# The first expert mixture in rounds of 416 moving tokens, with pieces of the weights stationary

## The reference

```python
x = attention(q, k, v)                         # local window of 16 and block summaries
# first mixture: two experts for each token
noisy = x @ w_gate + log1p(exp(x @ w_noise)) * noise
top2 = the two largest of noisy; top2_w = softmax over the two
for e in range(8):
    out[mask] += top2_w * (relu(x[mask] @ w1[e]) @ w2[e])
# second mixture: tokens with x @ w_skip > 0 get one expert; out = x + gate * expert(x)
```

## Time and profile before

| | us |
|---|---|
| median of 3 runs | 760.32 |
| lowest and highest | 758.58, 762.24 |
| the profiled execution | 759.18 |
| its span, from the first to the last instruction | 757.3 |
| PE busy with products and turns | 661.1 |
| DVE busy | 383.0 |
| ACT busy | 311.6 |
| POOL busy | 188.4 |

### The profile page before, as it was taken

The page is one execution under the profiler, slowest core; times in us unless marked ns, Lnnn a source line. Parts: engine busy times, 40 slices in busy tenths (PEclk is TensorE's granted clock), DMA queues, the critical chain, the costliest instruction groups (busy, mean ns, idle before and its releaser), DMA issues.

```text
span 757.3 us, 13865 instructions
## 1 busy us (share of the span) xinstructions
PE 661.1 (87%) x3940; PEld 533.5 (70%) x3940; DVE 383.0 (51%) x753; ACT 311.6 (41%) x512; POOL 188.4 (25%) x236
## 2 busy tenths in 40 slices
PE   5787884499999999999999999949399979999794
PEld 5676763387878878878788787836277768777583
DVE  2774787545454436254344363611655567447621
ACT  2364662144444334244343444414054465545511
POOL 1537750112222222222222222210012212212321
PEclk8898995599999999999999999988679998999997
DMA  9999993154656536447274456556436667557211
GB/s 196 212 223 250 247 345 115 32 161 128 177 130 176 129 88 163 99 125 181 43 181 125 99 156 150 155 121 189 119 129 185 210 217 232 174 173 251 41 41 15
DMA packets 94911, 117.12 MB, mean 155 GB/s; under 512 B 55380, under 2 KB 55508, under 8 KB 94864
## 3 DMA queue, kind: packets, MB, share of 16 engines
q1 hardware_dynamic: 77408, 91.10, 41.5%
q0 software_dynamic: 10528, 24.81, 17.2%
q10 hardware_dynamic: 6928, 0.66, 0.7%
HBM read 99.90 MB, written 20.98 MB: 160 GB/s over the span
## 4 chain that ended last, share of the span: by engine, by line
PE 61%; DMA 16%; SPq 8%; issue 6%; DVE 5%; POOLq 1%; ACT 1%; POOL 1%; ACTq 0%; DVEq 0%
PE bank L723 47%; DMA xg<-x_moe,ix_take 7%; DMA out<-y_sb,ix_put 6%; SPq L432 5%; PE bank L739 4%; PE bank L695 2%; SPq L447 2%; PE bank L644 1%; PE bank L622 1%; DVE col_val L1284 1%; PE bank L634 1%; PE bank L605 1%; PE bank L808 1%; DMA late_raw<-in_q 1%; PE bank L594 1%
## 5 line engine op out<-in xcount | busy, mean ns | idle before, releaser
L723 PE MATMUL bank<-w_hi,xt_hi 128*128 128x512 f32 x336 | 140.0, 417 | 16.1 <-DVE w_lo L1169 7.9
L1169 DVE TENSOR_TENSOR w_lo<-stage,w_hi x120 | 142.3, 1222 | 18.7 <-ACT w_hi L847 14.5
L1349 DVE TENSOR_TENSOR ht_lo<-bank,ht_hi 128x512 fp32r<-128x512 f32 x84 | 58.0, 691 | 168.2 <-ACT ht_hi L948 166.4
L723 PE MATMUL bank<-w_hi,ht_hi 128*128 128x512 f32 x336 | 139.7, 416 | 0.0
L723 PE MATMUL bank<-w_lo,xt_hi 128*128 128x512 f32 x336 | 135.1, 402 | 0.0
L723 PE MATMUL bank<-w_lo,ht_hi 128*128 128x512 f32 x336 | 131.8, 392 | 0.0
L847 ACT CAST w_hi<-stage x120 | 120.8, 1050 | 25.4 <-PEq L765 23.0
L945 ACT ACTIVATE h_sb<-bank 128x512 f32<-128x512 f32 x84 | 50.3, 598 | 113.5 <-PE bank L723 107.9
L723 PE MATMUL bank<-w_hi,xt_lo 128*128 128x512 f32 x336 | 93.1, 400 | 0.0
L948 ACT CAST ht_hi<-bank 128x512 fp32r<-128x512 f32 x84 | 49.3, 587 | 102.3 <-PE bank L739 102.3
L723 PE MATMUL bank<-w_hi,ht_lo 128*128 128x512 f32 x336 | 91.0, 393 | 0.0
(11 more groups left out here) (124 smaller groups left out, 703.7 us busy)
## 6 DMA issues: line engine op xcount, KB each, us to landing
stage<-in_moe_w SPq DMA_DIRECT2D x128, 512.0 KB
v_win<-in_v SPq DMA_DIRECT2D x24, 192.0 KB, 6.6
x_moe<-zeros SPq DMA_DIRECT2D x13, 260.0 KB, 4.1
x_att<-x_sb POOLq DMA_DIRECT2D x12, 256.0 KB, 5.2
x_sb<-x_moe SPq DMA_DIRECT2D x12, 256.0 KB, 2.7
out<-x_moe SPq DMA_DIRECT2D x4, 768.0 KB, 8.7
late_raw<-in_v SPq DMA_DIRECT2D x6, 384.0 KB, 7.3
stage<-in_k SPq DMA_DIRECT2D x6, 256.0 KB, 6.8
```

The source lines that it names most:

```text
L723: last = eng.matmul(ps[:], *every[i], start=(i == 0), stop=(i == len(every) - 1))
L1169: eng.tensor_tensor(piece(w_lo[n % SETS], j), stage[:, j, :], piece(w_hi[n % SETS], j).bitcast(F32), ALU.subtract)\
L1349: eng.tensor_tensor(ht_lo[:, half].rearrange("p k n -> p (k n)"), ps_ht[half][:], ht_hi[:, half].bitcast(F32).rearrange("p k n -> p (k n)" ...
```

## The change

The first mixture gets code of its own (`first_mixture` on each engine); the second keeps the slots (now `second_mixture`). The operands of the first change places: pieces of 128x128 of the weights are stationary, and the tokens, turned, move, up to 416 at a time. A *round* is 416 tokens of one expert in four parts of 128, 128, 128 and 32 rows, and with the counts above each expert has one round. The hidden layer comes out with the hidden units on the partitions, so that it needs no turn; the output comes out with its columns on the partitions and is turned back, in four chunks of 128 columns. The middle layer is made in two halves of four units of 128 ("units"); after each half its share of the output is added to four PSUM banks (`ps_out`). A round has 8 x 12 products for the units and 2 x 4 x 12 for the output. In the second half PE also turns the next round's x and, one chunk late, the output; the last chunk is turned behind unit 1 of the next round.

ACT has one instruction for a unit (relu and rounding at once), DVE one (relu of PSUM less the rounded part). POOL issues four gathers without waiting between them, PE waits for each by a semaphore of its own; and four scatters, whose landings are awaited together. A scatter leaves rows past the expert's count out, where they went to spare rows before. The table of pieces is `ROUND_PIECES`. `NBLK` grows from 12 to 16 (four rounds of four parts), with it `take_ix`, `put_ix`, `over` and `column_h` of both routings; the first routing has two more instructions, and the lists count rounds. Constants are loaded in two DMAs, and many tiles lie in other places: those of the routing, of the slots and of the rounds share memory.

```diff
+PART = (P, P, P, P // 4)
+PSTART = (0, P, 2 * P, 3 * P)
+W = sum(PART)
+PARTS = len(PART)
+ROUNDS = -(-N // W)
+NBLK = PARTS * ROUNDS
...
-SLOT_PIECES = ((2, 0, 1, 0), (2, 1, 2, 3))
+ROUND_PIECES = (0, 1, 0, 1, 0, 1, 0, 1, 1, 1, 1, 1)
+SLOT_PIECES = (2, 1, 2, 3)
...
+def block_starts(m):
+    b = np.arange(NBLK)
+    return b // PARTS * W + np.array(PSTART)[b % PARTS] if m == 0 else P * b
...
+            def first_mixture():
+                S = round_sems
+                eng.sem_inc(S["xtp"], 1)
+                def turn_x(n, t, ps):
+                    rows = PART[t]
+                    for i in range(DK):
+                        last = eng.transpose(ps[:, i * rows:(i + 1) * rows],
+                                             rows_in[0:rows, t, i * P:(i + 1) * P],
+                                             ident[0:rows, 0:rows])
+                    last.then_inc(S["xtp"], 1)
+                def turn_y(n, chunk):
+                    eng.wait_ge(S["yt"], n * DK + (chunk + 4))
+                    eng.wait_ge(S["ye"], n * DK + (chunk + 1))
+                    for t in range(PARTS):
+                        last = eng.transpose(ps_turn[0:PART[t], t * P:(t + 1) * P],
+                                             out_t[:, PSTART[t]:PSTART[t] + PART[t]], ident)
+                    last.then_inc(S["ytp"], 1)
+                def units(n, f, hi, lo):
+                    eng.wait_ge(S["hte"], n * FK + (f + 1))
+                    half, at = divmod(f * P, D)
+                    mine = [(w[:, FH * i + half, at:at + P], x[:, i, :])
+                            for x, ws in ((tok_hi, (hi, lo)), (tok_lo, (hi,)))
+                            for i in range(DK) for w in ws]
+                    for i, (w, x) in enumerate(mine):
+                        last = eng.matmul(ps_unit[f % 2][:, 0:W], w, x, start=(i == 0),
+                                          stop=(i == len(mine) - 1))
+                    last.then_inc(S["h"], 1)
+                def columns(f, chunk, hi, lo):
+                    for i, (w, h) in enumerate(((hi, unit_hi), (lo, unit_hi), (hi, unit_lo))):
+                        last = eng.matmul(ps_out[chunk][:, 0:W],
+                                          w[:, WC // 2 + f, chunk * P:(chunk + 1) * P],
+                                          h[:, f % UNITS, :], start=(f == 0 and i == 0),
+                                          stop=(f == FK - 1 and i == 2))
+                    return last
+                def one_round(e):
+                    hi, lo = w_hi[e % SETS], w_lo[e % SETS]
+                    n = eng.snap(number, min_val=0, max_val=E * ROUNDS)
+                    eng.wait_ge(S["xth"], n * PARTS + PARTS)
+                    eng.wait_ge(S["xte"], n * PARTS + (PARTS + 1))
+                    for part in range(FK // UNITS):
+                        mine = range(part * UNITS, (part + 1) * UNITS)
+                        for f in mine:
+                            units(n, f, hi, lo)
+                            if f == 1:
+                                turn_y(n, 0)
+                        if part == 0:
+                            if e == 0:
+                                eng.wait_ge(s_first, PIECES)
+                            else:
+                                eng.wait_ge(s_lo, PIECES * e)
+                        for chunk in range(DK):
+                            if part == 0:
+                                eng.wait_ge(S["yt"], n * DK + (chunk + 1))
+                            for i, f in enumerate(mine):
+                                if chunk == 0 and i >= UNITS - 2:
+                                    eng.wait_ge(S["hth"], n * FK + (f + 1))
+                                    eng.wait_ge(S["hte"], n * FK + (f + 3))
+                                if part and i == 2 and chunk:
+                                    turn_y(n, chunk)
+                                if part and i == 1:
+                                    eng.wait_ge(s_take[chunk], (n + 2) * 16)
+                                    eng.wait_ge(S["xte"], n * PARTS + (PARTS + chunk + 1))
+                                last = columns(f, chunk, hi, lo)
+                                if part and i == 1:
+                                    turn_x(n + 1, chunk, ps_x)
+                            if part:
+                                last.then_inc(S["y"], 1)
+                    eng.reg_add(number, number, 1)
+                    eng.reg_add(done, done, 1)
+                eng.wait_ge(s_route, 1)
+                eng.reg_load(counts, todo_i[0:1, 0:E])
+                for t in range(PARTS):
+                    eng.wait_ge(s_take[t], 16)
+                    turn_x(0, t, ps_out[t])
+                for e in range(E):
+                    if e == 0:
+                        eng.wait_ge(s_first, PIECES // 2)
+                    else:
+                        eng.wait_ge(s_lo, PIECES * e - PIECES // 2)
+                    eng.reg_mov(done, 0)
+                    with eng.While(lambda: eng.snap(done) < eng.snap(counts[e])):
+                        one_round(e)
+                    eng.drain().then_inc(s_wfree, 1)
+                turn_y(eng.snap(number, min_val=0, max_val=E * ROUNDS), 0)
...
+                def one_round(e):
+                    n = eng.snap(number, min_val=0, max_val=E * ROUNDS)
+                    for part in range(FK // UNITS):
+                        for f in range(part * UNITS, (part + 1) * UNITS):
+                            eng.wait_ge(S["h"], n * FK + (f + 1))
+                            eng.activation(unit_hi[:, f % UNITS, :], ps_unit[f % 2][:, 0:W], ACT.Relu)\
+                               .then_inc(S["hth"], 1)
+                            round_next(e + 1, f)
+                        for chunk in range(DK):
+                            if part == 0:
+                                round_next(e + 1, FK + chunk)
+                                continue
+                            round_x(n + 1, chunk, ps_x)
+                            eng.wait_ge(S["y"], n * DK + (chunk + 1))
+                            eng.wait_ge(S["ytp"], n * DK + (chunk + 1))
+                            eng.copy(out_t[:], ps_out[chunk][:, 0:W]).then_inc(S["yt"], 1)
...
+                def take(n, e, blocks):
+                    eng.wait_ge(S["xtp"], n * PARTS + 1)
+                    eng.sem_inc(S["start"], 1)
+                    eng.tensor_copy(ix_take[:], take_ix[:, e, blocks]).then_inc(S["ixt"], 1)
+                    eng.wait_ge(S["ixt"], n + 1)
+                    eng.wait_ge(S["gate"], n + 1)
+                    eng.sem_inc(S["start"], 1)
+                    for t in range(PARTS):
+                        rows = PART[t]
+                        eng.indirect_dma_start(rows_in[0:rows, t, :], None, x_dram,
+                                               bass.IndirectOffsetOnAxis(ap=ix_take[0:rows, t:t + 1],
+                                                                         axis=0),
+                                               bounds_check=N - 1).then_inc(s_take[t], 16)
+                def put():
+                    n = eng.snap(sent, min_val=0, max_val=E * ROUNDS)
+                    eng.wait_ge(S["ye"], n * DK + (DK + 2))
+                    eng.wait_ge(S["ix"], n + 1)
+                    eng.sem_inc(S["start"], 1)
+                    for t in range(PARTS):
+                        rows = PART[t]
+                        eng.indirect_dma_start(x1_dram,
+                                               bass.IndirectOffsetOnAxis(ap=ix_put[0:rows, t:t + 1],
+                                                                         axis=0),
+                                               rows_out[0:rows, t, :], None, bounds_check=N - 1,
+                                               oob_is_err=False, compute_op=ALU.add).then_inc(s_put[t], 16)
+                    for t in range(PARTS):
+                        eng.wait_ge(s_put[t], n * 16 + 16)
+                    eng.sem_inc(S["yfree"], 1)
...
+                        dv = eng.snap(done, min_val=0, max_val=ROUNDS - 1)
+                        take(round_now(), e, bass.ds(dv * PARTS, PARTS))
+                        with eng.If(round_now() >= 2):
+                            put()
...
+                if m == 0:
+                    eng.tensor_reduce(round_f[:, mine, tiles],
+                                      over[:, mine, tiles, PARTS - 1:NBLK - 1:PARTS], AX.X, ALU.add)
...
+                if m == 0:
+                    near = near_f
+                    then(eng.scalar_tensor_tensor(near_f[:, mine, tiles], round_f[:, mine, tiles],
+                                                  float(PARTS * P - W), rank_f[:, mine, tiles],
+                                                  ALU.mult, ALU.add))
...
-                then(eng.tensor_scalar(count_i[:], count[:], float(P - 1), None, ALU.add))
-                then(eng.tensor_scalar(nblk_i[:], count_i[:], 7, None, ALU.arith_shift_right))
+                if m == 0:
```

(104 more changed lines are left out.)

322 lines of the change are left out of this document (217 added, 105 removed).

## The result

The changed kernel takes 750.73 us, the median of 4 runs (747.26 to 752.08), and the kernel before 759.45 (757.31 to 762.24). The ratio is 0.9876 with a 95% interval of 0.9828 to 0.9924: faster by 1.2%, or 8.7 us. The forecast was 750, within 741 to 760, and 10.3 us less than before. The profiled execution took 752.08 us, with a span of 750.3.

What follows compares the result with a forecast made beforehand. PE at its upper clock was taken to bound the first mixture. PE's sequence -26.0, waits +5.2, head +4.3, tail +5.7 and second routing +0.5 gave -10.3 us: a median of 750 us, range 741 to 760.

Steps and rivals of the forecast that it cites:

- head: Before the first mixture: longer routing, four gather issues and a small last part delay PE's first product; +4.3 us.
- the wait at ps_x: Behind unit 7, DVE's queued work makes PE stand 0.65 us a round for that one buffer; +5.2 us in all.
- tail: Behind the first mixture's last product: last chunk's turns and scaling, then three scatters ahead of the last; +5.7 us.
- PE's sequence: First mixture on PE without new waits: 1536 products at 0.190 us plus turns, 327.7 us against 353.7; -26.0 us.
- rival (a): First mixture: weight load becomes the bound, no product faster than 0.22 us; 46 us on top, 796 us; 8%.
- point of decision: First mixture: from 0.1967 us a product on, the load-bound case decides, the forecast gain of 10.3 us being used up.
- Rival (b): First mixture: weight loads overlap no product, so 192 additional loads show 0.11 us each; 21 us more, 771 us; 2%.
- The expert's end: PE's stop between experts in the first mixture, carried over unchanged at 0.89 us for each of seven ends.
- The cover that held: Within rounds, one round of PE hides gather and scatter, some 7 and 11 us each if exposed; unit remainders in time.
- (c): Within a round, one covered item is late too, 1 us a round or so: 8 us, 758 us; 18%.
- (d): First mixture: each loop body's some 450 PE instructions run once; 762 us if each round lost 1.5 us; 4%.
- (e): More gain: 0.187 us a product with better overlapping scatters and gathers, or no ps_x wait; 741 to 745 us; 13%.

Runs made afterwards that it cites:

- the run of half products: Against the changed kernel, each middle-layer product of 416 columns issued as two of 208 with the same weights, each with its own load; 762.82 us, one run.

## Why the prediction was right, step by step

The terms, with what the two profiles show in their places (us):

| | forecast | profiles |
|---|---|---|
| up to the routing | 0 | -0.8 |
| head, from the routing to the first product | +4.3 | +5.3 |
| first mixture on PE, with the wait at ps_x | -20.8 | -21.1 |
| tail, to the last landing | +5.7 | +5.8 |
| from there to the second mixture | +0.5 | +0.4 |
| second mixture | 0 | +3.5 |
| sum (of unrounded terms) | -10.3 | -7.0 |

So the first mixture and what stands around it were forecast within 1.0 us a term. The second mixture was not; about 2 of its 3.5 us were that one execution. That the median lies within 0.7 us of 750 is in part luck: it fell by 8.7 us and not 10.3, and the kernel before was 0.9 faster in these runs than in those from which the forecast started.

**PE's sequence** (-26.0 forecast, -20.8 with the wait). The columns and a fixed part gave 0.190 us; the trace has 0.189, and the run with 404 columns 0.183 to 0.184. The groups of turns cost the 0.44 us that was carried over. The choice that mattered was to leave the weight load out as a bound; the run of half products shows what it is, 0.11 us, as the distance of the turns had said, and not the 0.19 of its record. So rival (a) would have been a misreading of a record, and its point of decision, 0.1967 us, was never near. Rival (b) is out by the pitch: if loads lay beside no product, one of 416 columns would take no less than 0.17 and 0.11, 0.28 us, and it takes 0.189. The sentence of the Trainium skill that was weighed there stands under "The mechanism" of "TensorE: Matmul & The Clock Gate", not under the heading that the prediction gives. The products here use all 128 rows, so by it no load would overlap, and this trace disagrees.

**The wait at ps_x** (+5.2). The mechanism was the one forecast, at its place, once a round: in the first round relu, piece, remainder, piece and the low part of x follow each other, `tok_lo` ends at 185.31, and PE starts its next product at 185.35, with the 0.53 us lost that its rows show. Taking the piece away from there gave 4.4 us, 0.55 a round where 0.65 stood in the sum.

**The expert's end** (0.89 each, carried over). It is the drain: 1.07 us with what follows it (7.5 / 7). Both kernels have it, so at most 0.18 us an end, 1.3 in all, came on top of what the forecast carried over. The smaller wait at ps_x and the product of 0.189 instead of 0.190 took that away again.

**The head** (+4.3). It was 5.3. The routing cost 1.1 us and not 1.8 (from its first instruction to the end of `take_ix` 18.23 us before, 19.37 after). The further issues on POOL follow each other by 1.43, 1.35 and 1.32 us from start to start, and not by 1.08 (the record leaves out 0.3 us of POOL's own between two):

```profile
142.22 1.13 POOL L1281 DMA_INDIRECT rows_in<-x_att,ix_take  x1 [1.01 <-POOL ix_take L1275]
...
145.00 1.01 POOL L1281 DMA_INDIRECT rows_in<-x_att,ix_take  x1 [0.30 <-issue]
...
146.32 0.94 POOL L1281 DMA_INDIRECT rows_in<-x_att,ix_take  x1 [0.30 <-issue]
```

But the chain hangs on the third gather, of 128 rows, not on the fourth: 2.8 us from the first, where 2.7 stood in the sum. That these two agree is luck: three issues of 1.08, less the half microsecond taken off for the small gather, come to nearly the same as two issues at their true distance. The mis-sized term is what follows the landing: 148.63 to 151.62, 3.0 us where I had put 1.7, since the third part's full turn (1.13 at half the clock) and rounding come before the small one's, with two gate copies between.

**The tail** (12.4 us from the last product to the last landing). It was 12.4, by two errors that cancel: luck, in this term. The issues lie 1.87 us apart (487.35 to 492.94 for three), not 1.6, and the last landing came 3.75 us behind its issue, not 4.4. The run with three scatters shows that the small one is covered by the third's landing.

**The cover that held.** The scatter within the rounds (no change with three instead of four), the gather, code that runs once (PE waits for nothing shown only at the seven drains), the remainders of units 2 and 3: rivals (c) and (d) have no wait in the trace. For (e), the head, the tail and 0.189 leave no room.

**Not forecast:** the second mixture's 26 products, at 0.234 instead of 0.229 us each by the addresses of its tiles. What that costs in time is too small for these runs; that it is small because most slots wait for DMAs is argued and not shown.

## What to carry to other kernels

Read the pitch of pipelined instructions from start to start, and the time for which a weight load holds PE from the shortest distance between two of them, not from their records; both decided the forecast of a change whose first rival would have been nearly 5% slower. After a change of shape, look again at the order of the small things around it: here a place in the table of pieces and a drain, neither of them needed where they stood, were worth 4.4 and 7.5 us of PE's time, more together than the 8.7 us of the change. Sums of a head and a tail can be right by errors that cancel, so test the parts: the fourth scatter, for which 1.9 us were expected, cost 0.1.

## What the hardware showed that I had not expected

The same products, with the same operand shapes and the same clock, took 5.94, 6.06 and 6.09 us for 26, by nothing but where the slots' tiles, the stationary tokens among them, lay in the partition: at their old addresses, 2944 bytes below and 2976 bytes below (worked out from the order in which the kernels take their memory). The weights lay 16384 bytes higher in the kernel before, which has 5.95, than in the run with the old addresses, which has 5.94, so their place is not it. The ten products of the second layer alone nearly keep their pace (2.32 and 2.33 us): it is the first layer's products, 0.227 or 0.234 us each. Which of the moved tiles and what rule of the addresses it is stay open; 32 bytes alone bring only 0.03 of the 0.15 us.

POOL needs nearly as long to issue an indirect DMA of 32 rows as one of 128: 0.94 us against 1.01 to 1.13 for a gather, 1.33 against 1.56 for a scatter.
